# Pooled attention with two expert layers on one core: ScalarE's exponential moved ahead of a copy in some steps, and the products with v dealt out anew

## What is computed

```python
# attention: B=4, H=8, S=1152, D=64, all float32
q_pool = q.reshape(B, H, S // 2, 2, D).mean(axis=3)          # 576 rows
scores = (1 / sqrt(D)) * q_pool @ k.T                        # 576 x 1152 per head
attn = exp(scores - max) / (sum + 1e-9)
x = attn @ v                                                 # then heads side by side: 2304 x 512
# soft mixture of 8 experts with 4 slots each, then x @ w_in -> g = h - tanh(h) -> g @ w_out
```

## Time and profile before

| | before |
|---|---|
| median of 3 runs | 929.97 us |
| profiled execution, its own time | 928.98 us |
| span in the trace | 927.1 us |
| TensorE matmuls busy | 859.4 us (93%) |
| TensorE weight loads busy | 622.0 us (67%) |
| VectorE busy | 559.1 us (60%) |
| ScalarE busy | 474.4 us (51%) |
| GpSimd busy | 432.7 us (47%) |
| mean granted clock of TensorE | 0.985 |

### The profile page before, as it was taken

The page is one execution under the profiler, slowest core; times in us unless marked ns, Lnnn a source line. Parts: engine busy times, 40 slices in busy tenths (PEclk is TensorE's granted clock), DMA queues, the critical chain, the costliest instruction groups (busy, mean ns, idle before and its releaser), DMA issues. The chain is left out here.

```text
span 927.1 us, 16086 instructions
## 1 busy us (share of the span) xinstructions
PE 859.4 (93%) x5499; PEld 622.0 (67%) x5499; DVE 559.1 (60%) x1165; ACT 474.4 (51%) x683; POOL 432.7 (47%) x277
## 2 busy tenths in 40 slices
PE   4899999999999999999999999878769999999998
PEld 3676776776666767766766766544225888888886
DVE  4676676676676666766666766350007666666763
ACT  3555455555555555555554554321009666666662
POOL 2845746746647548448448440000008644333343
PEclk9999999999999999999999999989879999999999
DMA  5443303303203113023033043408991000000000
GB/s 133 158 107 81 81 2 80 73 6 79 52 27 79 31 48 79 14 65 79 0 79 79 1 164 136 182 1 321 398 402 59 24 24 23 23 23 23 23 16 29
DMA packets 84208, 76.53 MB, mean 83 GB/s; under 512 B 42448, under 2 KB 62928, under 8 KB 83664
## 3 DMA queue, kind: packets, MB, share of 16 engines
q1 hardware_dynamic: 84176, 76.11, 26.0%
HBM read 71.37 MB, written 4.72 MB: 82 GB/s over the span
## 5 line engine op out<-in xcount | busy, mean ns | idle before, releaser
L590 ACT ACTIVATE prob<-ps,neg_max 128x1152 f32<-128x1152 f32 x144 | 175.4, 1218 | 75.7 <-DVE spare L542 75.7
L357 PE MATMUL ps<-ident,prob 128*128 128x128 f32 x1296 | 201.6, 283 | 10.6 <-ACT prob L590 7.8
L537 DVE TENSOR_REDUCE part_neg<-ps 128x1 f32<-128x512 f32 x288 | 186.2, 683 | 27.1 <-PE ps L341 26.7
L357 PEld LDWEIGHTS ps<-ident,prob 128*128 128x128 f32 x1296 | 143.3, 140 | 83.2 <-issue 36.6
L454 DVE COPY probT<-ps 128x512 f32<-128x512 f32 (+1 forms) x256 | 124.4, 486 | 120.1 <-PE ps L357 108.8
L341 PE MATMUL ps<-kT,qT_hi 128*128 128x512 f32 (+1 forms) x480 | 176.4, 385 | 6.1 <-DVE qT_lo L477 6.1
L601 ACT ACTIVATE probT<-ps 128x512 f32<-128x512 f32 x144 | 86.2, 599 | 158.3 <-PE ps L357 156.5
L374 PE MATMUL ps<-probT,v_nat 128*64 128x256 f32 (+1 forms) x1152 | 163.7, 415 | 1.1 <-DVE probT L452 1.0
L341 PE MATMUL ps<-kT,qT_lo 128*128 128x512 f32 (+1 forms) x480 | 159.7, 356 | 0.0
L217 POOL TENSOR_TENSOR qT_hi<-q_raw,ones 64x576 fp32r<-64x576 f32 x60 | 68.6, 1143 | 171.0 <-PE ps L341 144.2
L341 PEld LDWEIGHTS ps<-kT,qT_hi 128*128 128x128 f32 x480 | 94.3, 202 | 22.4 <-issue 12.2
(11 more groups left out here) (140 smaller groups left out, 1050.6 us busy)
## 6 DMA issues: line engine op xcount, KB each, us to landing
slot<-in_moe_w SPq DMA_DIRECT2D x16, 2048.0 KB, 13.4
k_nat<-in_k SPq DMA_DIRECT2D x32, 288.0 KB, 4.2
v_nat<-in_v SPq DMA_DIRECT2D x16, 576.0 KB, 4.7
q_nat<-in_q SPq DMA_DIRECT2D x32, 256.0 KB, 4.3
out<-res SPq DMA_DIRECT2D x18, 256.0 KB, 2.0
slot<-in_moe_w_in SPq DMA_DIRECT2D x2, 2048.0 KB, 21.5
slot<-in_moe_w_out SPq DMA_DIRECT2D x8, 512.0 KB, 17.1
q_nat_r<-in_q SPq DMA_DIRECT2D x32, 64.0 KB, 3.8
```

The lines of the kernel that those rows point to most:

```text
L357: last = nc.tensor.transpose(block_at(s, kt), src[:, kt * P:(kt + 1) * P], ident[:])
L537: nc.vector.tensor_reduce(part[:, c:c + 1], slot_banks(s)[:, c, :], AX.X, ALU.min).then_inc(part_done, 1)
L590: nc.scalar.activation(prob[prob_index(par, n)][:], slot_row(s), ACT.Exp, bias=neg_max[:, n:n + 1], scale=-1.0, accum_out=sums).then_inc(e ...
```

## The change

PV_STEPS moves products between steps: group 0 has 8, 6 and 4 products in the steps 8, 10 and 12 (it was 6, 8 and 4); group 1 has 4, 8 and 6 in the steps 14, 15 and 18 (it was 2, 8, 4 and 4 in 14, 15, 18 and 19). So the last product of group 1 runs one step earlier, and PV_LAST says 18 for it. OUT_STEP stays. In the steps named in EXP_FIRST, where the job of the step before is a T, ScalarE does the exponential first and then the copy of the transposed bank.

```diff
-    PV_STEPS = [{8: (0, 6), 10: (6, 14), 12: (14, 18)}, {14: (0, 2), 15: (2, 10), 18: (10, 14), 19: (14, 18)}]
-    PV_LAST = [12, 19]
+    PV_STEPS = [{8: (0, 8), 10: (8, 14), 12: (14, 18)}, {14: (0, 4), 15: (4, 12), 18: (12, 18)}]
+    PV_LAST = [12, 18]
     OUT_STEP = [14, 20]
+    EXP_FIRST = (0, 1, 8, 9, 10, 11)
...
                     t2 = job_at(s, 2, first, last)
-                    if t2 and t2[0] == "T":
-                        _, j, back = t2
-                        pp = p - back
-                        group_read(act, pp, j)
-                        act.wait_ge(ptr_full, (pp * TILES + j) * NCH + 1)
-                        evac_chunk(lambda d, s_: nc.scalar.activation(d, s_, ACT.Copy), s, j, 0).then_inc(first_evac, 1)
                     prev = job_at(s, 1, first, last)
-                    if prev:
-                        kind, n, back = prev
-                        t3 = job_at(s, 3, first, last)
-                        if kind != "T" and t3 and t3[0] == "T":
-                            wait(act, third_evac, (p - t3[2]) * TILES + t3[1] + 1)
-                        consume(kind, n, p - back, par ^ back, s - 1)
+
+                    def empty_bank():
+                        if t2 and t2[0] == "T":
+                            _, j, back = t2
+                            pp = p - back
+                            group_read(act, pp, j)
+                            act.wait_ge(ptr_full, (pp * TILES + j) * NCH + 1)
+                            evac_chunk(lambda d, s_: nc.scalar.activation(d, s_, ACT.Copy), s, j, 0).then_inc(first_evac, 1)
+
+                    def next_tile():
+                        if prev:
+                            kind, n, back = prev
+                            t3 = job_at(s, 3, first, last)
+                            if kind != "T" and t3 and t3[0] == "T":
+                                wait(act, third_evac, (p - t3[2]) * TILES + t3[1] + 1)
+                            consume(kind, n, p - back, par ^ back, s - 1)
+
+                    if s % STEPS in EXP_FIRST and prev and prev[0] == "T":
+                        next_tile()
+                        empty_bank()
+                    else:
+                        empty_bank()
+                        next_tile()
```

## The result

The changed kernel takes 924.73 us (median of 7 runs, 922.46 to 926.3), the kernel before 929.25 us in 7 runs; the ratio is 0.9943, with a 95% interval of 0.9924 to 0.9962. It is faster, but by 4.5 us where 16.7 were forecast, and 924.73 lies outside the range of 907 to 921. The times of different executions of one kernel lie some us apart; what of that the clock explains is told behind the experiments.

What follows compares the result with a forecast made beforehand. TensorE was taken as the bound, its matmuls busy 34.44 of 35.56 us per pair, plus small recurring waits. Savings of 0.62 + 0.11 + 0.17 + 0.20 = 1.10 us per pair, together 16.7, gave 913.3 us; range 907 to 921.

Steps and rivals of the forecast that it cites:

- (a): Steps 6 to 9: group 1's products end in step 6, step 8 takes 16 group 0 instructions; saves 0.62 us per pair.
- (b): Step 10 gives up four group 0 instructions, step 2 takes four of group 1; saves 0.11 us per pair.
- (c): Step 11: exponential first removes TensorE's stall of 0.33 us, but VectorE is late next; saves 0.17 per pair.
- (d): Step 1: exponential before the bank copy on ScalarE lets TensorE go on earlier; saves 0.20 us per pair.
- (e): Edits at nothing: step 0's swap is hidden behind products; steps 8, 9 and 10 swap nothing.
- Only the outT wait goes: Rival, chance 0.15: ScalarE's new order in steps 11 and 1 brings nothing; 0.73 us per pair, 919 us.
- Given back elsewhere: Rival, chance 0.07: T5's exponential in step 9 comes 0.6 us later, taking back the products' saving; 922 or 928 us.
- More than I say: Rival, chance 0.11: larger savings from products and exponential order, 1.49 us per pair; 907 us.
- Slower: Rival, chance 0.05: late maxima in steps 11 and 1 delay TensorE by one copy each; 937 us.
- The clock falls: Rival, chance 0.01: without products in step 7, TensorE's clock drops to 1.2 GHz there; 952 us.

Runs made afterwards that it cites:

- ninth_wait_late: Changed kernel, but products wait for VectorE's copies of the ninth blocks only ahead of the products that read them; 914.02 us, ratio to before 0.9818.
- late_wait_step8_twelve: ninth_wait_late with group 0's products dealt out as in the kernel before (12, 16 and 8 instructions in steps 8, 10, 12); 925.73 us, one run.
- late_wait_swap_1_only: ninth_wait_late with the exponential first in step 1 alone; 915.55 us, one run.
- order_only: Changed kernel's ScalarE order, with the products dealt out as in the kernel before; 928.46 us, ratio to before 0.9966.
- late_wait_swap_11_only: ninth_wait_late with the exponential first in step 11 alone; 918.48 us, one run.
- products_only: Products dealt out as in the changed kernel, with ScalarE's order as in the kernel before; 932.27 us, ratio to before 1.0023.
- before_ninth_wait_late: Kernel before, with only the later wait for VectorE's ninth-block copies added; 930.02 us, ratio to before 1.0008.

## Why the prediction was wrong, step by step

**The step that failed is (a)**, where it went from the transposes of outT to the products: "16 of group 0, 1.76 + 0.54 = 2.30", set down right behind them. The products have a wait of their own, for the copy of T4's ninth block. VectorE makes it only behind two reductions for T5, 3.2 after step 7. Before, this copy was hidden behind the wait for outT. I had looked for what is late next at the end of the chain (T5's exponential, 4.96) and not at each link of it. (a) was to save 0.62; it cost 0.10 (316.14 to 323.26 is 7.12, against 7.02), 0.72 a pair, 10.8 us in fifteen pairs. The value of 4.96 itself was right, as ninth_wait_late shows with 4.98, and late_wait_step8_twelve with a pair of 34.95.

**(b)** was forecast at 0.11 and is 0.15: step 10 with its products fell from 3.54 to 3.02 (325.55 to 328.57), step 2 grew from 3.22 to 3.59.

**(c)** was right in mechanism and nearly in size. Step 11 is 2.22, the ninth transpose of step 0 waits for VectorE, and steps 11 and 0 together give 0.22 (forecast 0.17, from 0.13 to 0.21, so just over). The full stall of 0.32 did not come off: VectorE's chain was indeed next.

**(d)** is 0.16, forecast 0.20. The copy does overlap the accumulator read, by 0.11 (336.08 against 336.19), but TensorE went on 0.15 after the copy's end and not 0.05. The Trainium skill (ScalarE: Activation LUTs, What ACT_TABLE_LOAD costs) puts the overlap of back-to-back ACTIVATEs at about 93 ns; the trace agrees, behind an accumulator read too.

**(e)** holds: step 0's swap is free, steps 8 to 10 swap nothing, the moved outT copy (317.71 to 318.10) ends before the copy of the bank can start at 318.29.

**What I left out of the sum** is two things. The first is the turn of the loop. Inside the loop every second pair was 0.09 longer in the kernel before and is about 0.29 longer now. Over the turn, step 0 starts 0.38 after the last score matmul of step 11, in the middle of the body 0.11 (330.79 less 330.68):

```profile
154.20 0.28 PE L342 MATMUL ps<-kT,qT_lo 128*128 128x128 f32 x1
154.58 1.09 PE L358 MATMUL ps<-ident,prob 128*128 128x128 f32 x8
```

Before, the wait for T7's exponential covered most of it: 0.52 over the turn, 0.44 in the middle. Where late_wait_swap_1_only brings that wait back, the turn costs 0.16 of a pair again and not 0.29. The loop makes six turns, so there are five such joints, and five times 0.20 are 1.0 us. The second is the second pair, where TensorE transposes a q that is only just loaded. GpSimd waits for this load until 54.80 before and until 54.74 in the changed kernel, and TensorE's transposes start at nearly the same time in the two (before, then changed):

```profile
56.62 0.63 PE L325 MATMUL ps<-ident,q_both 128*128 128x128 f32 x4 [0.15 <-POOL q_both_r L203]
```

```profile
56.56 0.63 PE L326 MATMUL ps<-ident,q_both 128*128 128x128 f32 x4 [0.60 <-ACT prob L591]
```

So this pair gained nothing (36.16 against 36.07), 0.5 us less than the others had. (The list names the exponential in the second row; GpSimd's work on q ends at 56.42.)

By these steps attention should be 16.7 - 10.8 - 1.0 - 0.5 + 0.6 (b) + 0.8 (c) - 0.6 (d) = 5.2 us shorter; by the table it is 5.4.

**The rivals.** *Only the outT wait goes* was wrong in both halves: the outT wait went and gave nothing, the order gave all. *Given back elsewhere* had the right shape, the gain of (a) gone, but named T5's exponential, which came when forecast, and argued from "nothing that the change moves"; the copy was not moved either, it was only uncovered. *More than I say* needed 0.80 in (a) and 0.33 in (c), and neither came. *Slower* did not come: T7's maximum is there at 328.56, 0.01 before step 11. *The clock falls* did not come either: in the changed kernel the granted clock is 1.00 from 17 to 588 us, all of attention. In that rival's text, that the clock fell "only" between 610 and 630 us is too strong: in the kernel before it is at 0.50 from 636 to 638 us too.

## What the runs showed that I had not expected

**The clock in the gating.** Behind attention, TensorE's granted clock falls from 2.4 to 1.2 GHz (1.00 to 0.50) for some us at a time, and at points that differ between the profiled executions. In windows of 2 us it is at 0.50 from 620 to 624 and from 636 to 638 in the kernel before, from 612 to 620 and from 626 to 634 in the changed kernel, and in order_only also from 592 to 600. From the first transposes of x to the first expert product it took 40.7 us in the kernel before (594.46 to 635.15), 43.6 in the changed kernel (588.88 to 632.49) and 44.8 in order_only (590.13 to 634.97). In order_only the clock fell within 2 us of the start. What TensorE did just ahead was the same as in the kernel before, which kept the full clock there: over 20 us matmuls are busy for 16.66 and 16.62, and these are the last 3 us in front of the first transposes of x, of the kernel before and of order_only:

```profile
591.46:594.46 3.00, 1.51 (x12) 0.74 (x9) 0.61 (x3) 0.38 (x1) 0.26 (x1) 1.00 1.00 407
```

```profile
587.13:590.13 3.00, 1.52 (x12) 0.74 (x9) 0.61 (x3) 0.38 (x1) 0.26 (x1) 1.00 1.02 419
```

And the same forty transposes in the two:

```profile
594.46 6.75 PE L699 MATMUL ps<-ident,x 128*128 128x128 f32 x40 [1.02 <-DVE unit L796]
```

```profile
590.13 9.69 PE L711 MATMUL ps<-ident,x 128*128 128x128 f32 x40 [1.01 <-DVE unit L808]
```

The window from 590 to 600 us has a granted clock of 0.58 in order_only:

```profile
590.00:600.00 10.00, 9.87 (x48) 6.69 (x52) 2.58 (x5) 2.60 (x4) 1.68 (x1) 0.58 0.09 36
```

The same stands in the other traces. Three profiled executions have a mean granted clock of 0.979 (order_only, late_wait_step8_twelve, late_wait_swap_11_only), and in all three these forty transposes take 9.5 to 9.8 us; in the nine others (0.983 to 0.987) they take 6.75. Of the runs without a trace only the time and the mean clock are on record, and the low clocks mostly go with the long times. Runs of one kernel lie up to 8 us apart (before 927.63 to 935.68, order_only 923.39 to 929.75), and medians don't add up.

Compared at the same mean granted clock (0.987 or more), the times follow attention: before 927.6 to 930.6, products_only 927.78, order_only 923.39 and 923.77, changed 922.46, ninth_wait_late 911.67 and 911.92. In the profiled executions the changed kernel gained 5.6 us by the end of attention, gave 2.9 back in the gating and gained 1.6 behind it: 4.3 in all, as the spans say. A mean clock of 0.981 or less came in four of 29 runs of the kernel before, in five of twelve of before_ninth_wait_late, seven of twelve of order_only and nine of twelve of products_only, but in none of seven of the changed kernel and none of six of ninth_wait_late. So the share is not the same for all kernels, and what in them makes the early fall likely stays open.

The Trainium skill (TensorE: Matmul & The Clock Gate, Part 4: PE-mode transpose) says that the full clock does not engage for transposes; here forty of them ran at a granted clock of 1.00 in the one execution and for the most part at half of it (0.58 in the mean) in the other, so the measurement speaks against it as a rule.

## What to carry to other kernels

When a wait is taken away, walk down the queue of the engine that waited, instruction by instruction, and write down for each next one what it waits for and when that is ready; a wait that is hidden today has no row in the list of waits. A semaphore wait that stands for a whole group ahead of its first instruction is worth splitting: moving it to the two products that need it turned a gain of 4.5 us into one of 15. Where, as in the gating here, the clock falls at points that vary from one execution to the next, compare steady pairs in the traces first, and medians only over many runs.
